# Softmax of a chunked attention: eight row-biased ScalarE exponentials in place of a VectorE centring, squares moved to ScalarE, two VectorE steps reordered

## The reference, cut to what is computed

```python
# chunked attention: 8 batches x 8 heads x 9 chunks of 64 rows, head size 64, all fp32
scores = scale * matmul(q_c, k_c.T)                  # 64 x 64 per chunk and head
scores = scores - max(scores, axis=-1)
attn = exp(scores); attn = attn / (sum(attn, axis=-1) + 1e-9)
x = matmul(attn, v_c)                                # 4608 tokens x 512
# dense layer
g = s * relu(x @ w_in) ** 2 + b                      # 512 -> 2048
x = g @ w_out                                        # 2048 -> 512
# routed layer: 8 experts, token computed if x @ w_skip > 0
e = argmax(x @ w_gate); y = gate * (relu(x @ w1[e]) @ w2[e]); out = x + y (or x)
```

## Time and profile before

| | |
|---|---|
| median of 3 runs | 1470.89 us (1470.71 to 1474.07) |
| the profiled execution | 1471.07 us, span 1469.3 us |
| mean granted PE clock | 0.973 |
| PE busy | 92% |
| PEld, DVE, ACT, POOL busy | 80%, 71%, 39%, 35% |

### The profile page before, as it was taken

One profiled execution on the slowest core, in us unless ns is written; L12 is line 12 of the kernel. 1 busy time (PEld: TensorE's weight loads), 2 busy tenths in 40 slices (PEclk: granted clock), 3 DMA queues, 4 the chain that ended last, 5 costly groups with the idle time before them and its releaser, 6 DMA issues.

```text
span 1469.3 us, 22247 instructions
## 1 busy us (share of the span) xinstructions
PE 1352.9 (92%) x7032; PEld 1179.3 (80%) x7033; DVE 1043.6 (71%) x2274; ACT 574.7 (39%) x1139; POOL 513.4 (35%) x454
## 2 busy tenths in 40 slices
PE   3799999999999999999999999999288889999998
PEld 3698888888888888888888888898267677888887
DVE  6684998979897989979898989956256745333332
ACT  4463444434343434434343444433054634222221
POOL 4342445344443434344443444323111212111111
PEclk8799999999999999999999999999599999999999
DMA  5232202112020202112021202032455841111110
GB/s 205 83 130 80 101 30 75 56 32 96 29 91 28 89 30 96 34 42 90 28 88 31 97 19 97 11 101 75 100 192 171 297 147 52 43 43 43 42 41 27
DMA packets 61436, 116.07 MB, mean 79 GB/s; under 512 B 11704, under 2 KB 20920, under 8 KB 61216
## 3 DMA queue, kind: packets, MB, share of 16 engines
q1 hardware_dynamic: 40816, 73.51, 15.3%
q10 hardware_dynamic: 14416, 27.79, 5.6%
q0 software_dynamic: 6112, 13.56, 2.8%
HBM read 90.49 MB, written 27.08 MB: 80 GB/s over the span
## 4 chain that ended last, share of the span: by engine, by line
PE 76%; DVE 9%; DMA 6%; issue 6%; ACT 1%; DVEq 1%; POOL 0%; ACTq 0%; SPq 0%; POOLq 0%
PE h_ps L601 25%; PE y_ps L615 23%; PE y_ps L719 9%; PE h_ps L706 8%; PE av_ps L582 4%; PE s_ps L564 3%; DMA wide<-x_rows,got 3%; DMA got<-table 2%; DVE rows_t_lo L967 1%; DMA table<-record,slot 1%; PE t_ps L699 1%; PE t_ps L572 1%; DVE g_lo L986 1%; PE av_ps L713 1%; DVE probs_t_lo L940 1%
## 5 line engine op out<-in xcount | busy, mean ns | idle before, releaser
L463 POOL TENSOR_TENSOR scratch<-scratch 128x384 f32<-128x384 f32 x192 | 186.0, 969 | 502.6 <-ACT scratch L815 502.5
L601 PE MATMUL h_ps<-rows_t_hi,weights_lo 128*128 128x384 f32 x768 | 261.3, 340 | 10.9 <-DVE rows_t_lo L967 5.8
L601 PE MATMUL h_ps<-rows_t_hi,weights_hi 128*128 128x384 f32 x768 | 260.6, 339 | 0.0
L601 PE MATMUL h_ps<-rows_t_lo,weights_hi 128*128 128x384 f32 x768 | 259.1, 337 | 0.0
L1007 DVE CUSTOM_DVE_ANT_0 products<-scratch,wide 128x512 f32<-128x512 f32 x297 | 238.3, 802 | 5.0
L815 ACT ACTIVATE scratch<-h_ps 128x384 f32<-128x384 f32 x192 | 94.5, 492 | 372.3 <-PE h_ps L601 368.6
L615 PE MATMUL y_ps<-weights_hi,g_lo 128*128 128x512 f32 x576 | 231.9, 403 | 0.0
L615 PE MATMUL y_ps<-weights_hi,g_hi 128*128 128x512 f32 x576 | 226.3, 393 | 0.0
L615 PE MATMUL y_ps<-weights_lo,g_hi 128*128 128x512 f32 x576 | 225.4, 391 | 0.0
L986 DVE TENSOR_TENSOR g_lo<-scratch,g_hi 128x384 fp32r<-128x384 f32 x192 | 141.2, 735 | 104.1 <-POOL scratch L463 82.0
L601 PEld LDWEIGHTS h_ps<-rows_t_hi,weights_lo 128*128 128x128 f32 x768 | 145.2, 189 | 24.6 <-DVE rows_t_lo L967 10.4
(11 more groups left out here) (147 smaller groups left out, 2509.4 us busy)
## 6 DMA issues: line engine op xcount, KB each, us to landing
qk_raw<-in_qk SPq DMA_DIRECT2D x66, 384.0 KB, 3.1
expert_raw<-in_w ACTq DMA_DIRECT2D x32, 512.0 KB, 5.0
scratch<-in_w ACTq DMA_DIRECT2D x21, 512.0 KB, 5.4
out<-scratch SPq DMA_DIRECT2D x12, 768.0 KB, 3.7
x_rows<-scratch SPq DMA_DIRECT2D x12, 768.0 KB, 5.2
v_raw<-in_v SPq DMA_DIRECT2D x66, 128.0 KB, 2.1
expert_raw<-in_w SPq DMA_DIRECT2D x11, 512.0 KB, 6.1
wide<-in_w_out SPq DMA_DIRECT2D x7, 512.0 KB, 4.6
```

What stands on the lines that cost most here:

```text
L463: pool.tensor_tensor(u_buf[f % 2], r_buf[f % 2], r_buf[f % 2], ALU.mult).then_inc(u_done, 1)
L601: mm = pe.matmul(h_ps[f % 2][:, 0:TOK], w[:, f // PAIR, kt, fs], x[:, z, kt, :], start=kt == 0 and n == 0, stop=kt == KT - 1 and n == 2)
```

## The change

Attention stage B: the subtraction of the row maximum and the row sum on DVE are gone. ACT first makes `row_bias` = -SCALE x row maximum (128x4), then runs eight exponentials, one for each half of the partitions and each of four heads, each 64 partitions x 64 columns, read from the scores in `s_ps`, with the bias of its rows as a per-partition operand and with the row sum as the accumulator output. PE's next scores wait for `exp_done` in place of `centered`. Squares: POOL's `squares` are gone; ACT computes the square into `u_buf` and then copies it to GH. Order on DVE: stages of one step in the order D, C, B, and `dots` stand ahead of B2.

```diff
@@ PE, stage B (and column_sums)
-                        pe.wait_ge(centered, n)
+                        pe.wait_ge(exp_done, n)
@@ POOL
-            def squares(i, f):
-                pool.wait_ge(r_done, FT * i + f + 1)
-                pool.tensor_tensor(u_buf[f % 2], r_buf[f % 2], r_buf[f % 2], ALU.mult).then_inc(u_done, 1)
@@ ACT, stage B
-                    act.wait_ge(centered, n + 1)
-                    act.activation(probs[:, c % 2, :, :], probs[:, c % 2, :, :], ACT.Exp, scale=SCALE).then_inc(exp_done, 1)
+                    act.wait_ge(max_done, n + 1)
+                    act.activation(row_bias[:, :], row_max[:, :], ACT.Copy, scale=-SCALE).then_inc(row_bias_done, 1)
+                    act.wait_ge(row_bias_done, n + 1)
+                    if not (isinstance(n, int) and n == 0):
+                        act.wait_ge(probs_done, n)
+                    for x in range(2):
+                        xs = slice(64 * x, 64 * x + 64)
+                        for h in range(4):
+                            last = act.activation(probs[xs, c % 2, h, :], s_blocks[xs, h, x, :], ACT.Exp,
+                                                  bias=row_bias[xs, h:h + 1], scale=SCALE, accum_out=row_sum[xs, h:h + 1])
+                    last.then_inc(exp_done, 1)
@@ ACT, hi_of_g
-                act.activation(GH[:, f % 2, :], r_buf[f % 2], ACT.Square).then_inc(g_hi, 1)
+                act.activation(u_buf[f % 2], r_buf[f % 2], ACT.Square).then_inc(u_done, 1)
+                act.wait_ge(u_done, FT * i + f + 1)
+                keep(GH[:, f % 2, :], u_buf[f % 2]).then_inc(g_hi, 1)
@@ DVE, stage B and B2
-                    dve.wait_ge(max_done, n + 1)
-                    for x, xs in enumerate(halves):
-                        m = row_max[xs, :].unsqueeze(2).broadcast_to([64, 4, CHUNK])
-                        last = dve.tensor_tensor(probs[xs, c % 2, :, :], s_blocks[xs, :, x, :], m, ALU.subtract)
-                    last.then_inc(centered, 1)
...
-                    dve.tensor_reduce(row_sum[:, :], probs[:, c % 2, :, :], AX.X, ALU.add).then_inc(sum_done, 1)
-                    dve.wait_ge(sum_done, n + 1)
@@ DVE, tile
-                        for stage, c in stages(f - 1):
+                        for stage, c in sorted(stages(f - 1), reverse=True):
                             attention(stage, CPT * (i + 1) + c, c, 1 - z)
                     lo_of_g(i, f)
                     if route and f == 0:
                         keep_x2(i - 1)
+                    if route and f < RANK_AT:
+                        dots(i - 1, DOTS_BY[f], DOTS_BY[f + 1])
                     if attend and f > 0:
                         for stage, c in stages(f - 1):
                             if stage == "B":
                                 attention("B2", CPT * (i + 1) + c, c, 1 - z)
-                    if route and f < RANK_AT:
-                        dots(i - 1, DOTS_BY[f], DOTS_BY[f + 1])
```

More of the change, by code:

```diff
@@ L103, in chunked_attention_moe @@
         row_inv = sb("row_inv", [P, 4], F32)
+        row_bias = sb("row_bias", [P, 4], F32)
         s_col = sb("s_col", [P, 1], F32)
@@ L226, in chunked_attention_moe @@
         max_done = sem("max_done")
-        centered = sem("centered")
+        row_bias_done = sem("row_bias_done")
         exp_done = sem("exp_done")
-        sum_done = sem("sum_done")
         eps_done = sem("eps_done")
@@ L487, in tile @@
             def tile(i, attend):
-                for f in range(FT):
-                    squares(i, f)
-                    for stage, c in stages(f - 1) if attend and f > 0 else ():
+                for f in range(1, FT) if attend else ():
+                    for stage, c in stages(f - 1):
                         if stage == "A":
@@ L512, in _ @@
             tile(0, True)
-            with pool.Fori(0, (TILES - 2) // 2) as two:
-                for z in range(2):
-                    i = two * 2 + 1 + z
+            with pool.Fori(1, TILES - 1, 2) as odd:
+                for i in (odd, odd + 1):
                     tile(i, True)
@@ L657, in column_sums @@
                 pe.wait_ge(raw_done, JOBS - EARLY)
-                pe.wait_ge(centered, 2 * CPT)
+                pe.wait_ge(exp_done, 2 * CPT)
                 pe.wait_ge(ones_set, 1)
@@ L982, in lo_of_g @@
             def lo_of_g(i, f):
-                dve.wait_ge(u_done, FT * i + f + 1)
                 dve.wait_ge(g_hi, FT * i + f + 1)
```

## The result

| | before | changed |
|---|---|---|
| median (lowest to highest), 4 runs each | 1472.26 us (1470.71 to 1474.07) | 1448.22 us (1446.48 to 1450.53) |
| profiled execution, its span | 1471.07, 1469.3 us | 1447.19, 1445.3 us |

The account below looks back on a forecast made before the run. The prediction took PE, busy for 92% of the span, as the bound. Body +7, tile 0 +5 and prologue +6 gave +18 us on 1471.07: 1489 us, range 1446 to 1540.

Parts of the forecast that it names:

- e = 3.2: ACT, stage B: the eight exponentials of a chunk together take 3.2 us, with bounds of 1.9 and 4.2.
- d = 0.40: ACT: the step from one exponential to the next takes 0.40 us, with accumulator read and no overlap, as on DVE.
- the prediction's own table: Whole kernel: forecast times for other exponential steps, from 1436 us at 0.24 to 1558 at 0.52.
- The loss and its size: Ten routed tiles: PE waits ahead of stage D cost 3.35 us a tile, 33.5 in all, against PE's pace of 10.02.
- the 3.35 us a tile can go: DVE order, C before B: low part of the probabilities comes at once, so PE's 3.35 us a tile can go.
- no one waits for POOL longer: Squares moved from POOL to ACT: POOL loses 192 instructions, and the move costs nothing while ACT is free.
- The ring, 7.7 + e: ACT and DVE wait for each other: a routed-tile chunk takes 7.7 + e = 10.9 us against PE's 10.02.
- Rival 1: ACT: accumulator read hidden, d up to 0.36, e at most 2.9, ring within PE's pace; 1436 to 1465 us; chance 0.32.
- Tile 0 and prologue, +5 and +6: Tile 0 loses 5 us through a longer ring; the prologue 6, as PE's next scores wait for the exponentials.
- 4.2 + e: Prologue: period of one chunk, 4.2 us plus the eight exponentials, 7.4 in place of 5.94.
- The rivals on the exponentials: Read hidden (1436 to 1465 us, chance 0.32), whole ACT instruction (1520 to 1558, 0.13), effects cancel (1467 to 1475, 0.09).
- the fourth: Routed tiles: stage D stalls stay because POOL's v_lo beside the dots makes DVE late; +30 us more; chance 0.02.

## Why the prediction was wrong in sign

**The exponentials, e = 3.2: the failed step.** The forecast took d = 0.40 for the step from one exponential to the next and e = 8d = 3.2 us for the eight. Measured were 2.60, d = 0.325 on average. This is the term that turned the sign: by the prediction's own table, 0.33 gives 1451 and a faster kernel, 0.37 no change and 0.40 the 1489. DVE's accumulator, from which I took the missing overlap, was the wrong model: on ACT the read of 0.19 starts 0.20 to 0.22 after its exponential and not behind it, and the next one starts 0.09 after the read. Against the kernel without reads (1.87 for eight) a read adds 0.09 an exponential, on average. At the step shown six steps are 0.29 to 0.31, and two are longer: 0.41 after the fourth (from 337.49 to 337.90), where the half of the partitions changes, and 0.42 from the eighth to the relu (338.78 to 339.20). What makes these two longer was not tried. The groups of ACT in the changed kernel:

```profile
L785 ACT ACTIVATE soft<-s_ps,row_bias 64x64 f32<-64x64 f32 x576 | 171.2, 303 | 3.2
L785 ACT ACTIVATION_READ_ACCUMULATOR soft<-s_ps,row_bias 64x1 f32 x576 | 111.3, 193 | 0.0
```

**The loss and its size: nearly right.** PE's own pace of 10.02 us a pair and 33.5 us in ten tiles: squares alone show 10.00 and 38.7. The sum of the prediction had left out the last pair of a tile's attention, 10.28 against 9.60.

**The DVE order, "the 3.35 us a tile can go": the wrong cause.** The stall had the order's place but DVE's load as its cause. The order alone gives 6 us of body, and in the changed kernel it costs 16. The prediction did have the 0.89 us of the low part in its ring, and did not ask what the ring would be without it.

**The squares, "no one waits for POOL longer", at nothing: the mechanism that was missed, though it did not move the sum.** They were worth 46 us alone and 52 in the changed kernel. The evidence was in the prediction: the multiply of 1.82 us beside POOL's 1.85 and 0.43 alone, a dot of 1.19. The prediction priced POOL's square by who waits for it, not by whom it slows. It used uncontended durations for the ring (0.73 a dot, 0.43 the multiply), which holds only because the squares go; with them on POOL the same kernel takes 1500 us. So the gain of the squares was in its numbers, under the order's name. That the sum is close for its e in spite of this is luck in part.

**The ring, 7.7 + e: right.** It measures 7.85 + 2.60, and ten exponentials give 11.04, 7.84 + 3.20. Rival 1, which came true in time and in d, had its mechanism half right: the accumulator's read is hidden in part, but the ring of 10.45 is longer than PE's pace, not within it, and at the 2.9 that the rival allowed it would have been 10.6.

**Tile 0 and prologue, +5 and +6: the prologue right, tile 0 short.** At 2.60 they came to +4.0 and +2.4 (the table by d had +2.5 and +3), at 3.20 to +7.7 and +5.9. The prologue's period, predicted as 4.2 + e, is 27.38 - 20.51 = 6.87:

```profile
20.51 0.55 PE L557 MATMUL s_ps<-qk_hi,qk_lo 128*128 128x256 f32 x1 [1.07 <-ACT soft L785]
...
27.38 0.55 PE L557 MATMUL s_ps<-qk_hi,qk_lo 128*128 128x256 f32 x1 [1.07 <-ACT soft L785]
```

**The tail and the experts, nothing: a gap.** They gave -5.9 and -1.8. POOL's queue in the last tile holds nothing but squares and record DMAs, and the DMAs come sooner although no one waited for a square. The experts' -1.8 is inside what the same code varies by, as said above.

**The sum.** With e at its measured size the prediction's own steps give about 1451, made of -25 + 5.5 on 1471; measured were -22.7 + 6.4 and the unforeseen -7.7. The rivals on the exponentials were the right question for the sign of the whole; the fourth asked about POOL beside the dots, and none asked what POOL's squares cost. What stays open: which of DVE's two order edits costs the 16 us, and the store's part in the tail.

## What to carry to other kernels

When an instruction of one kind takes two durations in a trace (0.43 and 1.82), find what runs beside the long ones before pricing any edit to that neighbour: work whose result is never late can be the most expensive in the kernel. If the long ones end a fixed time after the neighbour does, the two exclude each other. A stall's place shows which instruction is late, and not why; reordering moves it, and only less work on the late engine removes it. An edit made of several parts is worth running as its parts: here one of three carried twice the total, and the other two gave half of it back.

## What the runs showed of the hardware

- A two-input POOL multiply or subtraction in SBUF holds up DVE instructions that read two SBUF operands: a dot of 128x512 goes from 0.69 to 1.19 and 2.32 us, a low part of 128x384 from 0.56 to 1.88, a multiply of 128x256 from 0.43 to 1.82. The one that starts second ends its own time less 0.14 us after the first one's end (61 dots at 0.55, 42 multiplies at 0.28 in the kernel before), and POOL is held up by DVE in the same way (low part of v, 0.74 alone, 1.22). The addition of epsilon, which has one SBUF operand, is held up as well (0.17 to 0.35). DVE's maximum, which reads PSUM, and its row sum, which reads one SBUF operand, stay at 0.42 and 0.41.
- An accumulator output on ACT is an instruction of its own in the trace, 193 ns long on average, but costs 0.09 us net (eight exponentials: 1.87 us without, 2.60 with it).
- The granted clock that a trace gives for the prologue has to be read beside PE's pace. The table of stretches of before, then of the changed kernel (busy us of each engine, granted clock, DMA share, GB/s):

```profile
0.00:52.00 52.00, 21.14 (x84) 17.02 (x85) 33.85 (x73) 22.52 (x47) 25.30 (x31) 0.76 0.43 155
```

```profile
0.00:52.00 52.00, 21.53 (x81) 17.61 (x83) 19.00 (x53) 35.95 (x141) 23.59 (x31) 1.00 0.44 155
```

The trace of before has a clock record from 20.5 us on: until 58.0 it is 0.50 but for two stretches of 3.4 us at 1.00. PE's pace goes with it: matmuls of 256 columns start 0.21 us apart at 0.50 and 0.12 apart at 1.00 (from 23.43 and from 37.12), so the two levels, 1.2 and 2.4 GHz, show in the pace. The changed kernel's trace has no record before 58.8 us, and the table gives such a stretch as 1.00. Its matmuls there start 0.21 apart all through, the pace of the lower level, and those of `into_h` (384 columns) go from 0.32 to 0.18 apart at 58.8, where the record of 1.00 begins. `into_h` of step 0 takes 4.30 us in both (52.23 to 56.53, and 54.60 to 58.90). So the 1.00 of the changed kernel's prologue is a missing record, and not a higher clock.
